# Sorted rows read back in three transfers of two neighbours to a partition, and the first expert's gather placed 40 instructions ahead of a multiple of 256

## What is computed

```python
N, D, E, F = (768, 512, 8, 1024)            # tokens, width, experts, hidden
capacity = N // E * 2                       # 192
logits = x @ w_gate
expert_idx = np.argmax(logits, axis=1)
for i in range(N):                          # a token's place in its expert, in order
    e = expert_idx[i]
    if counts[e] < capacity:
        disp[e, counts[e]] = x[i]; pos[i] = counts[e]; counts[e] += 1; keep[i] = True
h = np.maximum(einsum('ecd,edf->ecf', disp, w1), 0.0)
y = einsum('ecf,efd->ecd', h, w2)
out[i] = gate_w[i] * y[expert_idx[i], pos[i]]
# then out goes through w_in, h * tanh(softplus(h)), w_out
```

## Time and profile before

| | us |
|---|---|
| median of 3 runs | 396.01 (395.2 to 396.07) |
| the profiled execution | 396.43 |
| its span, first to last instruction | 394.6 |
| TensorE busy with multiplies | 383.3 (97%) |
| VectorE / ScalarE / GpSimd busy | 282.0 / 233.5 / 115.9 |
| granted TensorE clock | 0.999 |

### The profile page before, as it was taken

How to read it: one execution, slowest core, us unless ns; L and a number is a source line. 1 busy time by engine, 2 the same in 40 slices (tenths; PEclk the granted TensorE clock), 3 DMA queues, 4 the chain that set the end, 5 groups by cost and what they waited for, 6 DMA issues and landing times.

```text
span 394.6 us, 6807 instructions
## 1 busy us (share of the span) xinstructions
PE 383.3 (97%) x2386; PEld 346.4 (88%) x2388; DVE 282.0 (71%) x446; ACT 233.5 (59%) x448; POOL 115.9 (29%) x122
## 2 busy tenths in 40 slices
PE   8999999999999999899999999999999999999995
PEld 3688999999999797889998999899899988999984
DVE  4888898899998626540447743569899998877861
ACT  5969869969887415630444654457666666544531
POOL 1853643742820060039999400000000000000015
PEclk9999999999999999999999999999999999999999
DMA  8684944973913347996797789091000000000004
GB/s 286 224 203 104 264 89 118 295 163 102 410 51 129 141 162 274 380 355 225 265 365 289 284 340 362 2 293 28 2 0 2 0 0 2 0 0 2 0 5 159
DMA packets 15804, 62.89 MB, mean 159 GB/s; under 512 B 2960, under 2 KB 3856, under 8 KB 11040
## 3 DMA queue, kind: packets, MB, share of 16 engines
q1 hardware_dynamic: 14272, 58.61, 44.2%
q0 software_dynamic: 992, 3.19, 2.1%
q10 hardware_dynamic: 512, 0.73, 0.6%
HBM read 49.89 MB, written 3.19 MB: 135 GB/s over the span
## 4 chain that ended last, share of the span: by engine, by line
PE 86%; ACT 4%; DVE 3%; DMA 3%; issue 2%; SPq 1%; POOLq 0%; POOL 0%; ACTq 0%; DVEq 0%
PE ps L1063 17%; PE ps L1088 16%; PE ps L938 14%; PE ps L983 9%; PE ps L832 7%; PE ps L860 7%; PE ps L730 7%; PE ps L1004 2%; DMA raw<-in_kt 2%; PE ps L687 2%; PE ps L914 1%; ACT prob L1170 1%; PE ps L803 1%; PE ps L964 1%; ACT pth L1216 1%
## 5 line engine op out<-in xcount | busy, mean ns | idle before, releaser
L938 PE MATMUL ps<-xs,ring 128*128 x512 | 60.8, 276 | 1.2 <-ACT xs L1259 1.0
L938 PEld LDWEIGHTS ps<-xs,ring 128*128 128x128 f32 x512 | 59.5, 191 | 2.0 <-issue 1.5
L1516 DVE TENSOR_TENSOR ptl<-ps,pth 128x384 fp32r<-128x384 f32 x96 | 49.0, 552 | 4.4 <-ACT pth L1216 3.8
L1216 ACT ACTIVATE pth<-ps 128x384 fp32r<-128x384 f32 x96 | 41.9, 490 | 16.1 <-PE ps L860 15.2
L1439 DVE TENSOR_REDUCE nmax<-ps 128x1 f32<-128x768 f32 x48 | 45.7, 955 | 5.2 <-PE ps L730 2.8
L662 POOL DMA_INDIRECT spare<-fold,toki x1 | 1.0, 1012 | 161.4 <-PE ps L1088 161.4
L730 PE MATMUL ps<-ops 128*128 128x384 f32 x192 | 44.3, 353 | 1.1 <-DMA ops<-qo 0.7
L1170 ACT ACTIVATE prob<-ps,nmax 128x768 f32<-128x768 f32 x48 | 43.4, 905 | 0.1
L1063 PE MATMUL ps<-yh,wih 128*128 128x384 f32 x128 | 43.0, 336 | 0.3 <-ACT yh L1281 0.3
L1063 PE MATMUL ps<-yh,wlow 128*128 128x384 f32 x128 | 42.8, 335 | 0.0
L1063 PE MATMUL ps<-yl,wih 128*128 128x384 f32 x128 | 41.9, 335 | 0.0
(11 more groups left out here) (193 smaller groups left out, 781.9 us busy)
## 6 DMA issues: line engine op xcount, KB each, us to landing
ring<-in_w SPq DMA_DIRECT2D x32, 1024.0 KB, 5.2
wraw<-in_w_in SPq DMA_DIRECT2D x2, 1280.0 KB, 8.3
wraw<-in_w_out SPq DMA_DIRECT2D x2, 1280.0 KB, 11.0
ops<-kh SPq DMA_DIRECT2D x12, 192.0 KB, 6.1
ops<-qh SPq DMA_DIRECT2D x6, 384.0 KB, 8.3
xg<-rows SPq DMA_DIRECT2D x1, 1539.0 KB, 6.3
raw<-in_vt SPq DMA_DIRECT2D x4, 384.0 KB, 5.4
wraw<-in_w_in SPq DMA_DIRECT2D x6, 256.0 KB, 5.0
```

Of the source, the lines that this page charges most:

```text
L938: last = mm(ps[:, fc // 2, (fc % 2) * WIDE:(fc % 2) * WIDE + W], wa[:, 2 * fc // KF, kd, P * (fc % (KF // 2)):P * (fc % (KF // 2)) + P], x ...
L1216: av(pth[:, (n // HT) % 2, HT * b:HT * b + HT, n % HT, :], ps[:, tile_banks(n)[b], 0:HALF].rearrange("p (a c) -> p a c", c=P), ACT.Copy).t ...
L1516: V.tensor_tensor(ptl[:, m2, HT * b:HT * b + HT, u, :], ps[:, tile_banks(n)[b], 0:HALF].rearrange("p (a c) -> p a c", c=P), pth[:, m2, HT ...
```

## The change

Three things are edited together.

1. The read-back is three transfers, g = 0, 2, 4. Each brings 256 sorted rows, two neighbours to a partition (4104 bytes): sorted row 128g+2p+t stands in partition p, place g+t. The first two transfers raise `back`, the third raises `back2`.
2. `rows_in` follows: TensorE waits for the first two transfers, transposes banks 0 to 3 (places 0 to 3), waits for the third and transposes banks 6 and 7. The copies into `xs` write at every second place, 8 bytes apart. The counts on `xa` and `xd` move with the order: all four groups of turn 1 now wait for the third copy of ScalarE or VectorE.
3. HEAD is 216: the gather begins 40 instructions ahead of a multiple of 256. The block pe_more (not run) needs 8 transposes where it had 24.

```diff
-        HEAD = 0
+        HEAD = 216
...
-        SHORT = WIDE // NT
+        NEAR = 2
+        SHORT = WIDE // NEAR
...
-        XT_BANKS = (SLOW, SLOW + 1, 0, 1, 2, 3)
+        XT_BANKS = (0, 1, 2, 3, SLOW, SLOW + 1)
+        FIRST_ROWS = 4
...
-        def by_slot(first_kd, end_kd, many):
-
-            return xs[:, first_kd:end_kd, 0:many].rearrange("q k (p t) -> q k t p", t=NT)
...
+        def near(ks, first_slot, slots):
+
+            return xs[:, ks, first_slot:first_slot + slots].rearrange("q k (g p t) -> q k g t p", g=slots // (NEAR * P), t=NEAR)
+
+        def many_slots(b):
+
+            if b >= SLOW:
+                return near(slice(2 * (b - SLOW), 2 * (b - SLOW) + 2), FIRST_ROWS * P, (NT - FIRST_ROWS) * P)[:, :, 0, :, :]
+            return near(slice(b, b + 1), 0, FIRST_ROWS * P)[:, 0, :, :, :]
...
-            sp.dma_start(xg[:, :, :], rows.rearrange("(p t) x -> p t x", t=NT)).then_inc(s["back"], 16)
+            for g in range(0, NT, NEAR):
+                sp.dma_start(xg[:, g:g + NEAR, :], rows[P * g:P * g + P * NEAR, :].rearrange(
+                    "(p t) x -> p t x", t=NEAR)).then_inc(s["back" if g < FIRST_ROWS else "back2"], 16)
...
-                    pe.wait_ge(s["back"], 16)
+                    pe.wait_ge(s["back"], 16 * FIRST_ROWS // NEAR)
                     for b in XT_BANKS:
+                        if b == SLOW:
+                            pe.wait_ge(s["back2"], 16)
...
-                            for t in range(NT):
+                            for t in range(NEAR):
                                 at = WIDE * (kd % 2) + SHORT * t
...
-                        if b == SLOW:
-                            av(by_slot(0, 2, T)[:, :, 4:NT, :], ps[:, b, :].rearrange("q (k t p) -> q k t p", k=2, p=P),
-                               ACT.Copy).then_inc(s["xa"], 1)
-                        else:
-                            av(by_slot(b, b + 1, T)[:, 0, 0:4, :], ps[:, b, :].rearrange("q (t p) -> q t p", p=P),
-                               ACT.Copy).then_inc(s["xa"], 2 if b == 0 else TURN * (E - 2) + 1)
+                        av(many_slots(b), many_tiles(b), ACT.Copy).then_inc(
+                            s["xa"], 1 if b < SLOW else TURN * (E - 2) + 2)
```

More of the change, by code:

```diff
@@ L260, in attention_moe_mish @@
                   "S", "max", "P", "T", "hi", "lo", "PV", "OT", "os", "om", "xw", "fw", "fr", "pa", "pd", "vs", "rc", "tiny",
-                  "g", "gex", "ohm", "lth", "gt", "gm", "gpos", "gst", "gkr", "hotr", "xga", "xgd", "perm", "tokc", "tokr", "si", "sc", "back", "wide", "xw0", "xw1", "xt", "xa", "xd",
+                  "g", "gex", "ohm", "lth", "gt", "gm", "gpos", "gst", "gkr", "hotr", "xga", "xgd", "perm", "tokc", "tokr", "si", "sc", "back", "back2", "wide", "xw0", "xw1", "xt", "xa", "xd",
                   "zy", "bnd", "Hw", "Ha", "Hd", "Yc", "Yw", "ya", "yd", "w2h", "w2l", "ye", "Ty",
@@ L333, in load_bounds @@
                 skip_runtime_bounds_check_because="starts and counts of T tokens, all written before the loop")[1]
-        SHORT = WIDE // NT
+        NEAR = 2
+        SHORT = WIDE // NEAR
         YB, YT, SLOW = 4, (5, 4), 6
         assert LAST_IN + 2 * NS + KF == 2 * KFF
-        XT_BANKS = (SLOW, SLOW + 1, 0, 1, 2, 3)
+        XT_BANKS = (0, 1, 2, 3, SLOW, SLOW + 1)
+        FIRST_ROWS = 4
+        assert FIRST_ROWS % NEAR == 0 and SHORT <= P
         def slot_in(f):
@@ L385, in xt_block, with many_tiles, wide_slots, wide_tiles @@
             return (2 * (b - SLOW) + i // 2, 4 + i % 2) if b >= SLOW else (b, i)
-        def by_slot(first_kd, end_kd, many):
-            return xs[:, first_kd:end_kd, 0:many].rearrange("q k (p t) -> q k t p", t=NT)
-        def by_tile(bank, ks, many):
-            return ps[:, bank, 0:ks * NT * many].rearrange("q (k t p) -> q k t p", k=ks, t=NT)
+        def near(ks, first_slot, slots):
[4 more added lines that the diff above has]
+            return near(slice(b, b + 1), 0, FIRST_ROWS * P)[:, 0, :, :, :]
+        def many_tiles(b):
+            return ps[:, b, :].rearrange("q (k t p) -> q k t p", k=2, p=P)
+        def wide_slots(ks):
+            return xs[:, ks, 0:WIDE].rearrange("q k (p t) -> q k t p", t=NEAR)
+        def wide_tiles(bank):
+            return ps[:, bank, 0:2 * WIDE].rearrange("q (k t p) -> q k t p", k=2, t=NEAR)
         def hold(e, passed, semaphore, value):
@@ L1306, in _ @@
                         act.wait_ge(s["wide"], 1)
-                        av(by_slot(0, 2, WIDE), by_tile(4, 2, SHORT), ACT.Copy).then_inc(s["xw0"], 1)
+                        av(wide_slots(slice(0, 2)), wide_tiles(4), ACT.Copy).then_inc(s["xw0"], 1)
                     with act.If(n_e > MIDDLE):
@@ L1587, in rows_in @@
                         dve.wait_ge(s["xt"], 2 * n + 2)
[L1588 to L1593, removed]
+                        V.tensor_copy(many_slots(b), many_tiles(b)).then_inc(
+                            s["xd"], 1 if b < SLOW else TURN * (E - 2) + 2)
                 def narrow():
@@ L1636, in _ @@
                         dve.wait_ge(s["wide"], 1)
-                        V.tensor_copy(by_slot(2, 4, WIDE), by_tile(5, 2, SHORT)).then_inc(s["xw1"], 1)
+                        V.tensor_copy(wide_slots(slice(2, 4)), wide_tiles(5)).then_inc(s["xw1"], 1)
                     with dve.If(n_e > MIDDLE):
```

## The result

| | before | after |
|---|---|---|
| median, us | 396.04 (395.1 to 396.55, 6 runs) | 401.22 (398.54 to 402.42, 6 runs) |
| profiled execution, us | 396.43 | 400.53 |
| its span, us | 394.6 | 398.7 |
| TensorE busy, us | 383.3 | 384.9 |
| turn 1's first multiply, us | 160.19 | 164.08 |

The ratio is 1.0125, 95% interval 1.0105 to 1.0145. The forecast was 395.7 with a range that ended at 396.7. The profiled execution explains 4.1 of the 5.2 us between the medians; it is one of the shorter runs of the changed kernel.

The account below looks back on a forecast made before the run. Scatter, read-back and first weight half were taken to set turn 1's first multiply, and so everything behind. Freed scatter -0.5 and three transfers +0.2 gave -0.3 us: median 396.01 to 395.7, range 394.7 to 396.7.

Parts of the forecast that it names:

- Part 1: HEAD's effect in turn 0: moved code packets free the scatter, -0.5 us; turn 0 ending 1.2 us earlier is worth 0.
- late code: At the branch into pe_narrow: code behind the gather's new crossing comes late, by 1.5 us; +0.9, 396.9; chance 0.10.
- What I called the code's wait: Turn 0's narrow body: TensorE's 0.15 us pause and ScalarE's hidden values 2.4 us late, both read as waiting for code.
- The scatter is freed: End of the scatter: without a code packet holding one DMA engine it lands up to 1.2 us earlier; taken as -0.5.
- The three transfers' price: Read-back: 384 pieces of 4104 bytes for 128 of 12312, at 167 ns each, cost +0.2 us.
- rival of small pieces: Read-back: pieces cost up to 310 ns, +3.1 us, 399.1; decides from 180 ns a piece; chance 0.05.
- The copies: Copies into xs ahead of turn 1: 8 bytes apart cost as unbroken ones, 598 and 692 ns; worth 0.
- wa0 sets turn 1: Start of turn 1: the first weight half, landing at 160.0, sets the first multiply at 160.19; copies would allow 159.6.
- rival of the lost straggler: Weights' stream: a code packet falls behind wa0, which lands at about 158.3; -1.0 us, 395.0; chance 0.17.
- passed on whole: Behind turn 1's first multiply: its shift of -0.3 us reaches the end of the kernel undiminished.
- The sum of -0.3 us: Turn 1's first multiply: -0.5 for the scatter and +0.2 for the transfers, giving a 395.7 median; chance 0.50.
- HEAD does nothing: Code fetched in blocks of 256 instructions is mostly hidden; supports the rival of a scatter not freed, 396.2, chance 0.18.

Follow-up runs that it names:

- the crossing at 139 and idle DMA engines: Changed kernel with the read-back and the weights behind it held until turn 0's second layer has first results; 401.58 us in one run.
- experiment 6: Kernel before the change, with GpSimd's scatter held until turn 0's first layer is done; 409.28 us in one run.
- HEAD 0: Changed kernel with HEAD back at 0, three transfers and new copies kept; 395.71 us, ratio 0.9990.
- the single transfer with HEAD 216: Kernel before the change with HEAD 216: unused block whole, 395.3 us, ratio 0.9989; block 32 instructions shorter, 400.43 us, ratio 1.0089.
- experiment 2: Here: kernel before the change, single transfer and old copies, with HEAD 216 and the unused block 32 instructions shorter; 400.43 us, ratio 1.0089.
- HEAD 232: Changed kernel with HEAD 232 for 216, crossing 123 instructions into the narrow body; 396.19 us, ratio 1.0016.
- HEAD 248: Changed kernel with HEAD 248 for 216, crossing 107 instructions into the narrow body, three transfers kept; 395.91 us, ratio 1.0008.
- HEAD 200: Changed kernel with HEAD 200 for 216, crossing 155 instructions into the narrow body; 400.48 us in four runs, ratio 1.0123.
- weights held: Changed kernel with only the next expert's weights held until turn 0's second layer is done, read-back left as it is; 399.35 us in one run.

## Why the prediction was wrong, point by point

- **The step that failed** is in Part 1: "With the crossing moved, the code packets should fall at about 142 and 148.2." The first did (142.50). For the second, 148.2 stands there without its working, 1.1 us ahead of the read-back's issue (149.3 in the same text), and it doesn't fit what the same part says just before: that the crossing comes 4 us later. The old packet moved at 146.7, and 4 us more are 150.7, behind the read-back's issue. With the crossing at 139 and idle DMA engines the packet came at 150.43; behind read-back and weights, at 157.38. So the step took for certain an overlap, fetch of code ahead of the bulk transfers, that its own numbers denied, and put its loss at nothing; it cost 3.54 us of idleness and 1.38 of slower transposes. I had the rows for it: the DMA engines are at their limit from there on the earlier trace rows, and I used that for the data and not for the code.
- **The rival "late code"** named the right mechanism at the wrong branch: the one into the narrow body, with at most 1.5 us at a place with 1.2 to spare. The branch that waited is the one out of it, where nothing is to spare but the 1.01 us ahead of turn 1. Its price was 5.55 us of branch, 3.5 of them seen, and 1.4 more for the slower clock. I had put 1.5 us on it and not asked what else the DMA engines carry when the code is fetched.
- **What I called the code's wait was two things.** TensorE's pause of 0.15 us at 147.00 went with the crossing, as said; but it is gone as well in experiment 6, where the crossing is that of before and only the scatter is moved, so the code alone doesn't make it. The 2.4 us of ScalarE's lateness did not, since they were never the code's. So turn 0 ended at 156.39 again and not at 155.2. Of the three marks in one place (pause, late values, code packet) only the packet is surely the code's.
- **The scatter is freed:** right, and by more. No packet moves from 147.65 to 149.5, where before had 5; the read-back is issued at 148.88, 0.95 earlier. From GpSimd's last issue to the read-back it takes 3.9 and 3.5 us in the two kernels whose code packet falls into the scatter (before, and after with HEAD 0) and 2.5 to 3.3 in the nine others whose read-back or scatter isn't held. In after itself the gain is lost again in the read-back, as the next point says.
- **The three transfers' price:** too low. The last part lands 7.2 us after the first issue (148.88 to 156.1) where the single one took 6.3, so +0.9 for my +0.2, and the 0.95 us by which the issue was earlier are used up. With HEAD 0 and 232 it is 7.2 and 7.5, against 6.7 and 6.8 for the single transfer with HEAD 216. From 152 to 154 us, for the earlier trace rows:

```profile
q1 hardware_dynamic: 150, 0.55, 76.1%
```

  0.55 MB are 134 pieces of 4104 bytes, and 76.1% of 32 us make some 182 ns for each, where I took 167 (half of all 384 took 160 or less, but the mean is 189). That is at the border of 180 from which the rival of small pieces was to decide, though not near its 310. And the engines stand idle for a quarter of the time, for which the sum had no term; why, no run shows. None of this made the slowdown (experiment 2).
- **The copies:** right. 631 to 642 ns and 691 to 694 for those 8 bytes apart, against 1156 and 1068:

```profile
L1276 ACT ACTIVATE xs<-ps x3: 631/632/642, 160.6 to 163.3; 128x512 f32<-128x512 f32 x3
L1605 DVE COPY xs<-ps x3: 691/692/694, 161.0 to 164.2; 128x512 f32<-128x512 f32 x3
```

- **wa0 sets turn 1:** right for before, wrong for what comes after it. Where no code is late, the first weights landed at 158.0 (HEAD 232) and 158.4 (HEAD 0), and ScalarE's third copy ended the wait, with turn 1 at 158.6 and 158.7, which is what the rival of the lost straggler looks like. With HEAD 248 they landed last (turn 1 at 160.37 after 1.25 us of waiting). Either way it is worth little. With HEAD 0 turn 1 starts 1.46 earlier and turn 2 0.66, but 0.69 of either lies ahead of the gather (135.67 for 136.36). Counted from the gather, turn 1 is 0.77 earlier and turn 2 0.03 later; in between, turn 1's second layer waits for VectorE's `hsl`. So "passed on whole" failed too: the shift of turn 1's first multiply didn't reach turn 2, and the median moved by 0.1.
- **The sum of -0.3 us** looks like what the edits give with HEAD 0 (395.71 against 395.85, ratio 0.9990), but that is luck: there the scatter isn't freed as the -0.5 wants it, and the transfers cost more than +0.2. With the scatter freed and the code in time the ratio is 1.0008 (HEAD 248) and 1.0016 (HEAD 232): no gain. The copies were priced rightly, the transfers some 0.7 us too low, and the forecast was 5 us off for the code packet whose new place I called free.
- The Trainium skill, "Runtime: NRT & Kernel Launch", Instruction fetch mechanics, says that the next block of code is fetched ahead and mostly hidden; I took it as speaking for "HEAD does nothing". The runs agree with the fetching ahead (150.4, well before the branch) and show where the hiding ends: the packet that moves at once on idle DMA engines moved 7 us later behind the data.

## What to carry to other kernels

When code moves by even a few dozen instructions, mark in the trace when the next block of code is fetched, and ask what the DMA engines are doing then and which jump out of the block comes next: here a bulk transfer issued just ahead of the fetch turned a hidden microsecond into a stall of 3.5 us, and TensorE, idle for so long, then ran its next work at the lower clock. An edit to a block that never runs did this (experiment 2), so each part of a change is to be tried at the same alignment before it is blamed. Three marks at one place in a trace are not one cause: hold the supposed cause back in a run and see which of them go.

## What the runs showed of the hardware

- A code packet of 16 KB moved at 150.43 us with idle DMA engines, at 153.96 behind a read-back of 1.5 MB, at 156.7 to 157.6 behind that and 2 MB of weights, and once, with the order changed, at 151.26 in their midst.
- From the end of that packet to the end of the branch that waited for it passed 1.37 us (after), 1.37 (experiment 2, the short block), 1.36 (HEAD 200) and 1.34 (weights held).
- After a hole of 3.5 us the granted clock was still 1.00 for the first 1.1 us of new work and then 0.50 (162.0 to 164.1). With HEAD 200, after a hole of 3.8 us, it was 0.50 from the first transpose (159.2 to 164.6), and the 24 took 5.39 us for 4.16 and 2.78. With its hole of 4.15 us experiment 2's took 4.42. So the slower clock cost 1.4 to 2.6 us beside the hole itself.
- TensorE's semaphores rose up to 3.5 us (before) and 2.4 us (after) behind the modelled end of their multiplies while GpSimd issued indirect transfers, and within 0.02 us in the one run in which these were moved away. The multiplies themselves were not slowed: 56 took 6.42 us with and without.
- Copies at 8-byte distance cost 632 ns (ScalarE) and 692 (VectorE) for 512 numbers, against 598 and 692 unbroken and 1156 and 1068 at 24 bytes.
